# First product of the first MLP by blocks: seven half-width products for eight, in two passes over the chunks

## Chip, cores and metric

One core of one Trainium2 chip. The metric is the device time of one execution in microseconds (us), lower is better. The kernel before ran three times: 810.62, 811.00 and 811.71, median 811.0.

## What is computed

Causal attention with a bias made of running sums, for 4 batches of 8 heads, 576 rows of 64; then two MLPs on 2304 tokens of width 512. All inputs and outputs are float32. The parts that matter here:

```python
x = attention(q, k, v, s)                  # (2304, 512)
h = x @ w_in                               # (2304, 2048)
g = h - np.tanh(h)
x = g @ w_out                              # (2304, 512)
h = x @ w2_in                              # (2304, 1024)
e = np.exp(h - max(h)); solu = h * e / sum(e)
ln = (solu - mean) / np.sqrt(var + 1e-06) * g_ln
out = ln @ w2_out                          # (2304, 512)
```

## The kernel before

Every operand of a matmul is split in a high part (rounded to float32r by ScalarE) and a low part (the rest, by VectorE or GpSimd); a product is three matmuls, high x high, high x low and low x high. Activations lie transposed in xT: features on the partitions, in four tiles kt of 128, tokens along the row. The stages follow each other: attention (16 pairs of heads, in a software pipeline over slots), the first MLP, the second MLP, and each begins while the last one ends.

The first MLP goes over five chunks of tokens: 512, 256 (the short one, c == 1), 512, 512 and 512. Each chunk goes through j = 0 to 15, the 128-wide tiles of the 2048 features. up (L1447) makes one tile of h in a PSUM bank with 4 kt x 3 = 12 matmuls as wide as the chunk; ScalarE takes tanh into gate (L847), VectorE subtracts it from the bank (L1141), ScalarE makes gate_hi (L860), VectorE gate_lo (L1153); down (L1459) adds the tile's part to four PSUM banks y_ps with 12 more matmuls. chunk (L1473) orders ups and downs on TensorE, a down two or four tiles behind its up. gate is a single buffer, gate_hi and gate_lo have two, so step (L843, L1137) waits for earlier downs. The first four ups stand inside the last slots of attention (first_up, L1489), and chunks 2 and 3 are a hardware loop. At a chunk's end copy_y (L977, L1275) brings the four banks to xT, and split_x (L806, L1101) splits the next chunk's x.

w_in and w_out stay in SBUF in both parts after chunk 0, where SP loads them tile by tile through the buffers stage (L549) and ScalarE and VectorE split them between the steps. In the last chunk the same is done for w2_in and w2_out: W2_STEP (L90) and W2O_STEP (L92) are written out by hand and say at which j each part is made, with GpSimd's four sums of w2_in's blocks (L701 to L710) before.

The second MLP already uses the scheme that the change brings to the first. Two token tiles and two halves of the features make a 2 x 2 block matrix; with the sums S1 to S4 of x's blocks and T1 to T4 of the weights' blocks, seven products (PRODUCTS, L94) in three PSUM banks give the four blocks that plain multiplication gives with eight. up2 (L1674) issues them, each 6 matmuls of 512 columns, and waits between them for keep and block_sum (L1296 to L1328), which add what has to be kept from bank to bank; ScalarE's copy_p1 (L1005) keeps the first product. GpSimd makes the sums and parts of x (split_y, L712). Then exp2, solu, moments, shift and normalise turn each row into ln, turn_ln transposes it, and down2 (L1725) multiplies by w2_out, whose parts w2o_hi and w2o_lo carry g_ln.

The order of work on every engine is the order of its program, written out by hand; semaphores count what is done. The end of the first MLP on TensorE is L1754 to L1758:

```python
chunk(NCH - 1, False)
up2(0, 0, 0, {})
down(NCH - 1, FT - 2, False)
down(NCH - 1, FT - 1, False)
up2(1, 1, 1, {4: (0, 0)})
```

## Time and profile before

| | |
|---|---|
| median of three runs | 811.0 us |
| the profiled execution | 810.19 us |
| its span on the core | 808.4 us |
| TensorE busy | 795.9 us, 98% |
| weight loads | 669.5 us, 83% |
| VectorE, ScalarE, GpSimd busy | 58%, 49%, 34% |
| granted TensorE clock | 1.00 |

The span runs from the first to the last instruction of the profile. Matmuls overlap, so the length shown of one (0.39 us at 512 columns) is more than the distance to the next; the distance between starts is what counts. PE is TensorE's matmuls, PEld its weight loads, DVE VectorE, ACT ScalarE, POOL GpSimd.

### The profile page before, as it was taken

The page shows a single profiled execution, that of the slowest core. Times are in us where ns is not written, and L with a number is a line of the kernel's source. Part 1 is how long each engine was busy: PE and PEld are TensorE (multiplying, and loading weights), DVE is VectorE, ACT ScalarE, POOL GpSimd, SP SyncE. Part 2 cuts the span into 40 slices and gives each one's busy share as a digit, 9 for nine tenths or more (in the row PEclk, how much of TensorE's full clock was granted, in tenths as well). Part 3 has the DMA queues.
Part 4 walks back from the last instruction along what each step waited for, and adds up shares of the span by engine and source line. Part 5 has one row for each costly group of instructions (what it writes and reads, how often), then busy time and mean ns, then how long its engine had stood idle before and what let it go on. Part 6 is the DMA issues. An engine that isn't in the chain of part 4 may idle for free. (4 is left out here: it accounts for less than half of the span.)

```text
span 808.4 us, 14647 instructions
## 1 busy us (share of the span) xinstructions
PE 795.9 (98%) x4532; PEld 669.5 (83%) x4532; DVE 465.7 (58%) x1101; ACT 395.9 (49%) x935; POOL 273.7 (34%) x322
## 2 busy tenths in 40 slices
PE   7999999999999999999999999999999999999998
PEld 6888888887888899988888888888887788888886
DVE  5889899897954342422233222453668666666661
ACT  5999999997643232322223222443344344433342
POOL 3778877877100000000000000016553754444400
PEclk9999999999999999999999999999999999999999
DMA  7656556553523200000000000002000000000001
GB/s 182 165 150 157 142 151 160 151 139 115 156 95 103 79 1 1 1 1 1 1 0 0 0 0 0 1 1 104 1 1 0 27 27 27 26 25 14 25 14 53
DMA packets 77723, 46.40 MB, mean 57 GB/s; under 512 B 59824, under 2 KB 68144, under 8 KB 77680
## 3 DMA queue, kind: packets, MB, share of 16 engines
q1 hardware_dynamic: 75232, 45.19, 19.8%
q10 hardware_dynamic: 2448, 0.66, 0.4%
q8 instruction: 24, 0.39, 0.2%
q14 instruction: 19, 0.16, 0.1%
HBM read 40.97 MB, written 4.87 MB: 57 GB/s over the span
## 5 line engine op out<-in xcount | busy, mean ns | idle before, releaser
L1455 PE MATMUL psum<-x_hi,w1i 128*128 128x512 f32 (+1 forms) x640 | 181.9, 369 | 0.5 <-issue 0.5
L1468 PE MATMUL psum<-gate_hi,w1o 128*128 128x512 f32 (+1 forms) x640 | 146.0, 370 | 0.0
L1455 PEld LDWEIGHTS psum<-x_hi,w1i 128*128 128x128 f32 x640 | 115.4, 188 | 21.3 <-issue 0.7
L1468 PEld LDWEIGHTS psum<-gate_hi,w1o 128*128 128x128 f32 x640 | 112.4, 188 | 21.1
L1153 DVE TENSOR_TENSOR gate_lo<-gate,gate_hi 128x512 fp32r<-128x512 f32 (+1 forms) x80 | 53.6, 670 | 125.0 <-ACT gate_hi L860 125.0
L1455 PE MATMUL psum<-x_lo,w1i 128*128 128x512 f32 (+1 forms) x320 | 117.7, 368 | 0.0
L702 POOL TENSOR_TENSOR w2t<-stage 128x512 f32<-128x512 f32 x2 | 4.3, 2154 | 327.9 <-DVE w2x L1127 327.9
L860 ACT ACTIVATE gate_hi<-gate 128x512 fp32r<-128x512 f32 (+1 forms) x80 | 47.2, 590 | 134.6 <-PE psum L1468 126.4
L1141 DVE TENSOR_TENSOR gate<-psum,gate 128x512 f32<-128x512 f32 (+1 forms) x80 | 51.0, 638 | 95.8 <-ACT gate L847 94.2
L847 ACT ACTIVATE gate<-psum 128x512 f32<-128x512 f32 (+1 forms) x80 | 44.4, 555 | 111.8 <-PE psum L1455 90.8
L885 ACT ACTIVATE probs<-probs,neg_max 128x128 f32<-128x128 f32 (+2 forms) x144 | 83.6, 586 | 9.9 <-DVE neg_max L1186 9.7
L1169 DVE TENSOR_TENSOR pT_lo<-psum,pT_hi 128x512 fp32r<-128x512 f32 (+3 forms) x160 | 72.5, 478 | 12.1 <-ACT pT_hi L876 10.7
L1468 PE MATMUL psum<-gate_lo,w1o 128*128 128x512 f32 (+1 forms) x320 | 79.2, 369 | 0.0
L876 ACT ACTIVATE pT_hi<-psum 128x512 fp32r<-128x512 f32 (+3 forms) x160 | 64.1, 434 | 10.4 <-PE psum L1590 9.9
L1455 PEld LDWEIGHTS psum<-x_lo,w1i 128*128 128x128 f32 x320 | 60.2, 188 | 10.1
L1738 PE MATMUL psum<-w2o_a,lnT_hi 128*128 128x512 f32 x216 | 67.8, 395 | 0.3 <-DVE lnT_lo L1379 0.3
L1468 PEld LDWEIGHTS psum<-gate_lo,w1o 128*128 128x128 f32 x320 | 56.9, 189 | 11.1
L1186 DVE CUSTOM_DVE_ANT_0 probs<-psum,cum_bc 128x128 f32<-128x128 f32 (+3 forms) x128 | 58.5, 481 | 11.2 <-PE psum L1518 8.8
L1590 PE MATMUL psum<-ident,probs 128*128 128x128 f32 x400 | 57.9, 275 | 1.0 <-DVE pT_lo L1169 0.5
L1557 PE MATMUL psum<-pT_hi,v_parts 128*128 128x128 f32 (+2 forms) x192 | 56.1, 330 | 0.5 <-DVE pT_lo L1169 0.5
L1705 PE MATMUL psum<-w2x,y_split_a 128*128 128x512 f32 x210 | 50.8, 396 | 0.0
L1557 PE MATMUL psum<-pT_lo,v_parts 128*128 128x128 f32 (+2 forms) x192 | 48.3, 311 | 0.0
(158 smaller groups left out, 1408.5 us busy)
## 6 DMA issues: line engine op xcount, KB each, us to landing
cum_bc<-cum_dram SPq DMA_DIRECT2D x16, 576.0 KB, 4.7
rden_T<-rden_dram SPq DMA_DIRECT2D x32, 144.0 KB, 3.1
out_x<-out_sb SPq DMA_DIRECT2D x18, 256.0 KB, 2.0
stage<-in_q SPq DMA_DIRECT2D x32, 128.0 KB, 2.6
v_raw<-in_v SPq DMA_DIRECT2D x32, 128.0 KB, 3.7
stage<-in_moe_w_in SPq DMA_DIRECT2D x16, 256.0 KB, 3.0
stage<-in_moe_w_out SPq DMA_DIRECT2D x16, 256.0 KB, 3.3
stage<-in_k SPq DMA_DIRECT2D x28, 128.0 KB, 2.3
```

Of the source, the lines that this page charges most:

```text
L876: hi = act.activation(to(pT_hi), ps, ACT.Copy)
L885: act.activation(probs[par][:, at:at + width], probs[par][:, at:at + width], ACT.Exp, bias=neg_max[par][:, col:col + 1], scale=-1.0, accum ...
L1141: dve.tensor_tensor(gate[:, 0:n], h_ps[j % 4][:, 0:n], gate[:, 0:n], ALU.subtract).then_inc(gate_done, 1)
L1153: dve.tensor_tensor(gate_lo[j % 2][:, 0:n], gate[:, 0:n], gate_hi[j % 2][:, 0:n].bitcast(F32), ALU.subtract).then_inc(gate_lo_done, 1)
L1169: lo = dve.tensor_tensor(to(pT_lo), ps, to(pT_hi).bitcast(F32), ALU.subtract)
L1186: dve.tensor_tensor_reduce(probs[par][:, at:at + width], tail_bank(sl) if h is None else score_ps[h][t], cum_tail[:, :] if h is None else ...
L1455: mm = pe.matmul(h_ps[j % 4][:, 0:wide(c)], wp[j][:, kt, :], xp[:, kt, 0:wide(c)], start=(n == 0), stop=(n == 3 * KT - 1))
L1468: mm = pe.matmul(y_ps[m][:, 0:wide(c)], wp[j][:, m * P:(m + 1) * P], gp[j % 2][:, 0:wide(c)], start=(j == 0 and wp is w1o_hi and gp is gat ...
L1557: mm = pe.matmul(x_ps[:, c0:c1], v_parts[par][:, j, 2 * h * D:2 * h * D + P], pp[:, h, j * STEP + c0:j * STEP + c1], start=(j == 0 and n = ...
L1590: mm = pe.transpose(ps[:, n * P:(n + 1) * P], probs[par][:, at:at + P], ident[:, :])
L1705: mm = pe.matmul(h2_ps[n][at], yp[:, of, kt, :], wp[:, kt, :], start=(nth == at and kt == 0 and k == 0), stop=(last and kt == HK - 1 and k ...
L1738: mm = pe.matmul(out_ps[par], lp[par][:, f, :], wp[f][:, :], start=(f == 0 and n == 0), stop=(f == FT2 - 1 and n == 2))
```

## The change

The first MLP runs over half of h (8 of the 16 tiles j, FT1) at a time. CHUNKS lists the passes: chunks 0, 1, 2, 3, 4 with the first half, then 4, 0, 1, 2, 3 with the second. The first pass over chunk 0 is computed as before (8 ups, 8 downs). The other nine runs are 36 groups: a group g is a run and a pair of tiles j, four pairs a run, 28 on full chunks and 8 on the short one (runs 0 and 6). Tokens of the chunk in two halves, features in two halves and the pair's two tiles make the blocks, and products (new) issues seven products of 6 matmuls, each half a chunk wide (n, 256 columns or 128), in banks 0 to 2, with the weights' block as the stationary operand; before it was 24 matmuls of the full width. downs is the old down for the pair's two halves of the gate, one group later.

Beside it: ScalarE copies product 1 and C11 out of PSUM, VectorE adds five block sums per group to h_blocks in SBUF (block_sum1), the tanh and the gate now read h_blocks; before a new chunk seven blocks of x are summed (GpSimd), rounded (ScalarE) and their low parts taken (GpSimd three, VectorE four); each weight pair takes four sums (pair_sums, GpSimd), three copies (pair_hi, 512, 256 and 1024 wide) and three low parts (pair_lo), for the second half in groups 13 to 16, with w_out's in 14 to 17. y of the first pass goes to y_half and by DMA to y_dram, and comes back to be added by GpSimd (add_y); only chunk 4 stays. w2_in is split in the last two groups, w2_out at the start of the second MLP. split_y has 10 instructions in place of 12.

```diff
+    FT1 = FT // 2
+    CHUNKS = [0, 1, 2, 3, 4, 4, 0, 1, 2, 3]
...
+    PAIRS1 = FT1 // 2
+    GROUPS = PAIRS1 * (len(CHUNKS) - 1)
+    LAST_GROUP = GROUPS - 1
...
+        def group(g):
+            run, pair = divmod(g, PAIRS1)
+            return run, pair, wide(CHUNKS[run + 1]) // 2
+        SPLIT_RUNS = [run for run in range(len(CHUNKS) - 1) if CHUNKS[run + 1] != CHUNKS[run]]
+        def ahead_of(g):
+            run, pair = divmod(g + 1, PAIRS1)
+            return run if pair == 0 and run in SPLIT_RUNS else None
+        def x_free(eng, run, name):
+            if run == 0:
+                eng.wait_ge(up_done, FT1 if XB_AT[name] > 2 else AHEAD)
+            else:
+                eng.wait_ge(pair_product, 7 * (PAIRS1 * run - 1) + XB_AT[name] + 1)
...
+            c = CHUNKS[e]
+            return y_half[:, m, 0:wide(c)] if e < NCH else xT[:, m, tokens(c)]
...
+            def store_half(e):
+                sp.wait_ge(y_act, 2 * (e + 1))
+                sp.wait_ge(y_dve, 2 * (e + 1))
+                n = wide(CHUNKS[e])
+                sp.dma_start(y_dram[CHUNKS[e], :, :, 0:n], y_half[:, :, 0:n]).then_inc(y_stored, 16)
...
+                sp.wait_ge(w1i_lo_done, FT1 - 3 + n)
+                sp.wait_ge(w1o_lo_done, FT1 - 3 + n)
+                load_pair(n)
...
+            def pair_sums(n):
...
+                pair_free(pool, n)
+                pool.tensor_tensor(t1, b12, b11, ALU.subtract).then_inc(w1b_summed, 1)
+                pool.tensor_tensor(t3, b22, b12, ALU.subtract).then_inc(w1b_summed, 1)
+                pool.wait_ge(w1b_summed, 4 * n + 1)
+                pool.tensor_tensor(t2, b22, t1, ALU.subtract).then_inc(w1b_summed, 1)
+                pool.wait_ge(w1b_summed, 4 * n + 3)
+                pool.tensor_tensor(t4, b21, t2, ALU.subtract).then_inc(w1b_summed, 1)
...
+            def x_low(run, name):
+                pool.wait_ge(xb_hi_done, 7 * SPLIT_RUNS.index(run) + XB_HI.index(name) + 1)
+                pool.tensor_tensor(x_part(run, name, 1), x_block(run, name), x_part(run, name, 0).bitcast(F32),
+                                   ALU.subtract).then_inc(xb_low_pool, 1)
+            def split_blocks(run):
+                x_low(run, "A11")
+                x_sums(run, XB_SUM)
+                x_low(run, "A12")
+                x_low(run, "A22")
...
-            pool.wait_ge(y_act, 2 * (NCH - 1))
-            pool.wait_ge(y_dve, 2 * (NCH - 1))
-            pool.wait_ge(down_done, FT * (NCH - 1) + 10)
+            pool.wait_ge(x_done, PAIRS)
+            x_sums(0, XB_SUM[:2])
+            pair_sums(0)
+            x_low(0, "A11")
+            pair_sums(1)
+            pair_sums(2)
+            x_sums(0, XB_SUM[2:])
+            x_low(0, "A12")
+            x_low(0, "A22")
+            pair_sums(3)
+            for run in (1, 2, 3):
+                split_blocks(run)
+            for n in range(PAIRS1, 2 * PAIRS1):
+                pair_sums(n)
+            split_blocks(5)
+            add_y(5)
+            split_blocks(6)
+            add_y(6)
+            split_blocks(7)
+            add_y(7)
...
-            pool.wait_ge(up_done, FT * NCH)
+            w2_sums("T1", LAST_GROUP - 2)
+            add_y(8)
+            w2_sums("T2", LAST_GROUP - 1)
+            w2_sums("T4", LAST_GROUP - 1)
...
-            pool.wait_ge(y_act, 2 * NCH)
-            pool.wait_ge(y_dve, 2 * NCH)
...
+            def pair_hi(n):
...
+                hi = w1b[n % PAIRS1][:, 0, :, :, :]
+                pair_free(act, n)
+                act.activation(hi[:, 0:2, :, :], first.rearrange("p (b k) f -> p b k f", b=2), ACT.Copy).then_inc(w1b_hi_done, 1)
+                act.activation(hi[:, 2, :, :], second[:, HK:KT, :], ACT.Copy).then_inc(w1b_hi_done, 1)
+                act.wait_ge(w1b_summed, 4 * (n + 1))
+                act.activation(hi[:, 3:7, :, :], w1b_raw[n % PAIRS1][:, 1, 3:7, :, :], ACT.Copy).then_inc(w1b_hi_done, 1)
...
+                        act.wait_ge(w2_in[kt], 16)
...
+            def copy_first(g):
+                run, pair, n = group(g)
+                act.wait_ge(pair_product, 7 * g + 1)
+                act.wait_ge(gate_done, FT1 + 2 * g)
+                act.activation(h_blocks[:, 1, 0:n], h1_ps[0][:, 0:n], ACT.Copy).then_inc(first_copied, 1)
+            def copy_c11(g):
+                run, pair, n = group(g)
+                act.wait_ge(pair_product, 7 * g + 4)
+                act.activation(h_blocks[:, 0, 0:n], h1_ps[0][:, 0:n], ACT.Copy).then_inc(c11_copied, 1)
+            def tanh(g, t):
+                run, pair, n = group(g)
+                act.wait_ge(block_summed, 5 * g + 4 + t)
+                if t == 1:
+                    act.wait_ge(c11_copied, g + 1)
+                act.wait_ge(gate_lo_done, FT1 + 2 * g + t)
+                act.activation(gate_pair(gate, n), h_pair(t, n), ACT.Tanh).then_inc(tanh_done, 1)
+            def gate_high(g, t):
+                run, pair, n = group(g)
+                u = FT1 + 2 * g + t
                 act.wait_ge(gate_done, u + 1)
...
-                act.activation(gate_hi[j % 2][:, 0:wide(c)], gate[:, 0:wide(c)], ACT.Copy).then_inc(gate_hi_done, 1)
-                if isinstance(c, int) and c == 0 and 0 < j <= FT - AHEAD:
...
+            for g in range(GROUPS):
+                run, pair, n = group(g)
+                ahead = ahead_of(g)
+                copy_first(g)
+                if pair == 1:
+                    copy_y(run)
+                if ahead is not None:
+                    x_hi_part(ahead, "A11")
+                copy_c11(g)
+                if ahead is not None:
+                    x_hi_part(ahead, "S1")
+                if g == 0:
+                    pair_hi(PAIRS1 - 1)
+                if 0 <= g - 3 * PAIRS1 - 1 < PAIRS1:
+                    pair_hi(PAIRS1 + g - 3 * PAIRS1 - 1)
+                if 0 <= g - 3 * PAIRS1 - 2 < PAIRS1:
+                    for j in range(2):
+                        w1o_hi_later(2 * (g - 3 * PAIRS1 - 2) + j)
+                if g == LAST_GROUP - 1:
+                    w2i_hi_part("T1")
+                    w2i_hi_part("T2")
+                    w2i_hi_part("T4")
+                if g == LAST_GROUP:
+                    w2i_hi_part("B11")
+                tanh(g, 0)
+                if ahead is not None:
+                    for name in XB_HI[2:]:
+                        x_hi_part(ahead, name)
+                if g == LAST_GROUP:
+                    w2i_hi_part("B21")
+                    w2i_hi_part("B22")
+                gate_high(g, 0)
+                tanh(g, 1)
+                if g == LAST_GROUP:
...
             def copy_p1(i, n):
                 act.wait_ge(product_done, 7 * i + 1)
                 if isinstance(i, int) and i == 0:
-                    act.wait_ge(w2o_lo_done, 2)
...
+                    act.wait_ge(w2_summed, 4 * HK)
+                    act.wait_ge(w2i_lo_done, 7)
                 wait(act, ln_step, 18 * same_banks(i) - 7)
                 act.activation(h_sums[n][0], h2_ps[n][0], ACT.Copy).then_inc(p1_copied, 1)
...
             copy_p1(0, 0)
+            for f in range(4):
+                w2o_hi_part(f)
             exp2(0, 0, 0)
+            w2o_hi_part(4)
+            w2o_hi_part(5)
             exp2(0, 1, 0)
-            copy_y(NCH - 1)
+            copy_y(len(CHUNKS) - 1)
             normalise(0, 0)
+            w2o_hi_part(6)
+            w2o_hi_part(7)
             copy_p1(1, 1)
...
+            def block_sum1(g, product, at, block):
+                run, pair, n = group(g)
+                dve.wait_ge(pair_product, 7 * g + product)
+                kept = h_blocks[:, 1, 0:n] if block in (1, 2, 3) and product < 4 else h_blocks[:, block, 0:n]
+                dve.tensor_tensor(h_blocks[:, block, 0:n], h1_ps[at][:, 0:n], kept, ALU.add).then_inc(block_summed, 1)
+            def keep_first(g, product, at, block):
+                dve.wait_ge(first_copied, g + 1)
+                block_sum1(g, product, at, block)
...
+            def gate_of(g, t):
+                run, pair, n = group(g)
+                dve.wait_ge(tanh_done, FT1 + 2 * g + t + 1)
+                dve.tensor_tensor(gate_pair(gate, n), h_pair(t, n), gate_pair(gate, n), ALU.subtract).then_inc(gate_done, 1)
...
+            for g in range(GROUPS):
+                run, pair, n = group(g)
+                ahead = ahead_of(g)
+                if pair == 1:
+                    copy_y(run, 2)
+                keep_first(g, 2, 1, 2)
+                keep_first(g, 3, 2, 3)
+                if pair == 1:
+                    copy_y(run, 3)
+                if g == LAST_GROUP - 1:
+                    w2i_lo_part("T1")
+                dve.wait_ge(block_summed, 5 * g + 2)
+                block_sum1(g, 5, 1, 3)
+                block_sum1(g, 6, 2, 2)
+                block_sum1(g, 7, 1, 1)
+                gate_of(g, 0)
+                if ahead is not None:
+                    for name in XB_SUM[:3]:
+                        x_low_sum(ahead, name)
+                if g == LAST_GROUP - 1:
+                    w2i_lo_part("T2")
+                if g == LAST_GROUP:
+                    w2i_lo_part("B11")
+                gate_low(FT1 + 2 * g, 2 * n)
+                if ahead is not None:
+                    x_low_sum(ahead, XB_SUM[3])
+                if g == 0:
+                    pair_lo(PAIRS1 - 1)
+                if 0 <= g - 3 * PAIRS1 - 1 < PAIRS1:
+                    pair_lo(PAIRS1 + g - 3 * PAIRS1 - 1)
+                if g == LAST_GROUP - 1:
+                    w2i_lo_part("T4")
+                if g == LAST_GROUP:
+                    w2i_lo_part("B21")
+                gate_of(g, 1)
+                if 0 <= g - 3 * PAIRS1 - 2 < PAIRS1:
+                    for j in range(2):
+                        w1o_lo_later(2 * (g - 3 * PAIRS1 - 2) + j)
+                if g == LAST_GROUP:
+                    w2i_lo_part("B22")
...
             keep(0, 0)
+            w2o_lo_part(0)
+            w2o_lo_part(1)
             c11(0, 0)
             c22(0, 0)
             c12(0, 0)
             row_max(0, 0)
             c21(0, 0)
             row_max(0, 1)
+            w2o_lo_part(2)
+            w2o_lo_part(3)
             solu(0, 0, 0)
             moments(0, 0)
-            copy_y(NCH - 1)
+            w2o_lo_part(4)
+            w2o_lo_part(5)
+            copy_y(len(CHUNKS) - 1, 2)
+            copy_y(len(CHUNKS) - 1, 3)
             shift(0, 0)
             solu(0, 1, 0)
             keep(1, 1)
             moments(0, 1)
+            w2o_lo_part(6)
...
+            def products(g):
+                run, pair, n = group(g)
+                if run in (0, NCH - 1):
...
+                for nth, (rows, columns, at) in enumerate(PRODUCTS):
+                    if pair == 0 and run in SPLIT_RUNS:
+                        if rows in XB_SUM:
+                            pe.wait_ge(xb_low_dve, 4 * SPLIT_RUNS.index(run) + XB_SUM.index(rows) + 1)
+                        else:
+                            pe.wait_ge(xb_low_pool, 3 * SPLIT_RUNS.index(run) + XB_LOW.index(rows) + 1)
+                    if g == 0 and nth < 3:
+                        pe.wait_ge(gate_done, AHEAD + nth + 1)
+                    elif nth == 0:
+                        pe.wait_ge(c11_copied, g)
+                    elif nth < 3:
+                        pe.wait_ge(block_summed, 5 * g)
+                    elif nth == 3:
+                        pe.wait_ge(first_copied, g + 1)
+                    elif nth < 6:
+                        pe.wait_ge(block_summed, 5 * g + nth - 3)
+                    else:
+                        pe.wait_ge(block_summed, 5 * g + 3)
+                    last = nth == max(k for k, p in enumerate(PRODUCTS) if p[2] == at)
+                    for kt in range(HK):
+                        for k, (xp, wp) in enumerate(((0, hi), (0, lo), (1, hi))):
+                            mm = pe.matmul(h1_ps[at][:, 0:n], wp[:, W1B_AT[columns], kt, :],
+                                           x_blocks[:, XB_AT[rows], xp, kt, 0:n],
+                                           start=(nth == at and kt == 0 and k == 0), stop=(last and kt == HK - 1 and k == 2),
+                                           skip_group_check=True)
+                    mm.then_inc(pair_product, 1)
+            def downs(g):
+                run, pair, n = group(g)
...
+                    pe.wait_ge(y_act, 2 * (run + 1))
+                    pe.wait_ge(y_dve, 2 * (run + 1))
+                for t in range(2):
+                    if run == NCH - 1:
+                        pe.wait_ge(w1o_lo_done, FT1 + 2 * pair + t + 1)
+                    down(FT1 + 2 * g + t, 2 * pair + t, pair == 0 and t == 0, pair == PAIRS1 - 1 and t == 1, 2 * n)
             def first_up(j):
...
+                first_down(j)
+            products(0)
+            first_down(FT1 - 1)
+            for g in range(1, GROUPS):
+                products(g)
+                downs(g - 1)
...
             up2(0, 0, 0, {})
-            down(NCH - 1, FT - 2, False)
-            down(NCH - 1, FT - 1, False)
+            downs(LAST_GROUP)
             up2(1, 1, 1, {4: (0, 0)})
```

## Rows read from the trace of the kernel before

**Rows 1.** The page: busy time, share of the span, instructions.
```profile
PE 795.9 (98%) x4532; PEld 669.5 (83%) x4532; DVE 465.7 (58%) x1101; ACT 395.9 (49%) x935; POOL 273.7 (34%) x322
```
**Rows 2.** Chunks 2 to 4: length, busy PE, PEld, DVE, ACT, POOL; PEclk, DMA, GB/s.
```profile
336.83:580.00 243.17, 243.17 (x1066) 199.69 (x1065) 84.33 (x117) 72.93 (x115) 21.55 (x14) 1.00 0.03 9
```
**Rows 3.** Timeline (start us, length us): first matmuls of ups, chunks 0 and 1.
```profile
222.62 0.62 PE L1455 MATMUL psum<-x_hi,w1i 128*128 128x512 f32 x2
...
228.11 0.62 PE L1455 MATMUL psum<-x_hi,w1i 128*128 128x512 f32 x2
...
299.79 0.40 PE L1455 MATMUL psum<-x_hi,w1i 128*128 128x256 f32 x2
...
302.64 0.40 PE L1455 MATMUL psum<-x_hi,w1i 128*128 128x256 f32 x2
```
**Rows 4.** Timeline, TensorE: narrow matmuls in attention, transposes in the second MLP.
```profile
186.86 0.25 PE L1557 MATMUL psum<-pT_hi,v_parts 128*128 128x192 f32 x1
...
187.22 0.55 PE L1590 MATMUL psum<-ident,probs 128*128 128x128 f32 x3
...
616.85 1.03 PE L1721 MATMUL psum<-ident,act 128*128 128x128 f32 x8
617.64 3.25 PE L1705 MATMUL psum<-w2x,y_split_b 128*128 128x512 f32 x12
```
**Rows 5.** Timeline, weight loads beside the same matmuls of attention.
```profile
186.97 0.19 PEld L1557 LDWEIGHTS psum<-pT_hi,v_parts 128*128 128x128 f32 x1
187.08 0.19 PEld L1557 LDWEIGHTS psum<-pT_lo,v_parts 128*128 128x128 f32 x1
```
**Rows 6.** Timeline: from TensorE to VectorE and from VectorE to TensorE.
```profile
594.77 9.96 PE L1705 MATMUL psum<-w2x,y_split_a 128*128 128x512 f32 x42
...
597.84 0.69 DVE L1301 TENSOR_TENSOR stage<-psum,stage 128x512 f32<-128x512 f32 x1 [0.57 <-PE psum L1705]
...
189.47 0.69 DVE L1169 TENSOR_TENSOR pT_lo<-psum,pT_hi 128x512 fp32r<-128x512 f32 x1
...
190.31 0.56 PE L1557 MATMUL psum<-pT_hi,v_parts 128*128 128x128 f32 x2 [0.54 <-DVE pT_lo L1169]
```
**Rows 7.** Groups of instructions by form, and two rows of the timeline (they begin with a time).
```profile
L847 ACT ACTIVATE gate<-psum 128x512 f32<-128x512 f32 x64 | 38.3, 598 | 98.3 <-PE psum L1455 78.4 <-DVE gate_lo L1153 19.9
...
L980 ACT ACTIVATE xT<-psum 128x256 f32<-128x256 f32 x2 | 0.7, 381 | 0.3 <-PE psum L1468 0.3
...
L825 ACT ACTIVATE w2x<-w2t 128x1024 fp32r<-128x1024 f32 x4 | 4.2, 1050 | 0.0
...
L832 ACT ACTIVATE w2x<-stage 128x512 fp32r<-128x512 f32 x6 | 7.0, 1214 | 0.0
...
L1141 DVE TENSOR_TENSOR gate<-psum,gate 128x256 f32<-128x256 f32 x16 | 6.8, 424 | 13.0 <-ACT gate L847 13.0
...
L1127 DVE TENSOR_TENSOR w2x<-stage,w2x 128x512 fp32r<-128x512 f32 x6 | 6.6, 1158 | 4.6 <-ACT w2x L832 4.6
...
L1133 DVE SCALAR_TENSOR_TENSOR w2o_a<-stage,g_col,w2o_a 128x512 fp32r<-128x512 f32 x6 | 4.5, 804 | 0.0
...
L734 POOL TENSOR_TENSOR y_split_b<-y_sum,y_split_b 128x512 fp32r<-128x512 f32 x4 | 5.2, 1297 | 0.7 <-POOL y_split_b L731 0.7
...
560.83 1.22 DVE L1122 TENSOR_TENSOR w2x<-w2t,w2x 128x1024 fp32r<-128x1024 f32 x1 [0.26 <-ACT w2x L825]
...
245.52 0.69 DVE L1153 TENSOR_TENSOR gate_lo<-gate,gate_hi 128x512 fp32r<-128x512 f32 x1 [2.79 <-ACT gate_hi L860]
```
**Rows 8.** Timeline, VectorE's gate_lo while GpSimd forms w2_in's sums (542.5 to 558.1).
```profile
542.50 4.28 POOL L702 TENSOR_TENSOR w2t<-stage 128x512 f32<-128x512 f32 x2 [327.91 <-DVE w2x L1127]
...
546.26 1.07 DVE L1153 TENSOR_TENSOR gate_lo<-gate,gate_hi 128x512 fp32r<-128x512 f32 x1 [1.91 <-ACT gate_hi L860]
...
551.75 0.86 DVE L1153 TENSOR_TENSOR gate_lo<-gate,gate_hi 128x512 fp32r<-128x512 f32 x1 [2.17 <-ACT gate_hi L860]
...
557.24 1.39 DVE L1153 TENSOR_TENSOR gate_lo<-gate,gate_hi 128x512 fp32r<-128x512 f32 x1 [2.17 <-ACT gate_hi L860]
```

559 lines of the change are left out of this document (338 added, 221 removed).

## The prediction

> **What bounds the kernel now.** I read the page first: TensorE is busy for 98% of the span [rows 1]. Then the table of stretches: in the steady chunks of the first MLP it is busy in every microsecond, while ScalarE and VectorE work a third of the time and GpSimd hardly at all [rows 2]. So here the time is the pitch of the matmuls, and I took that from the timeline: 24 matmuls of 512 columns from 222.62 to 228.11, 5.49 us or 0.2288 each; 24 of 256 columns from 299.79 to 302.64, 2.85 us or 0.1188 each [rows 3]. A line through both is 0.0088 us + 0.00043 us per column. Then I asked what a matmul costs whose columns are few: in attention four of 192, 192, 64 and 64 columns take 0.36 us where the line gives 0.25, and the eight 128-column transposes take 0.79, where it gives 0.51 [rows 4]; the weight loads beside them follow each other at 0.11 [rows 5]. Weights in 32 bits seem to need 0.11 us each, and 256 columns just cover that.
>
> **Matmuls removed and added.** For a pair of feature tiles the first product was 24 matmuls of a chunk's width; now it is 42 of half that width. A group on a full chunk: 24 x 0.2288 = 5.49 becomes 42 x 0.1188 = 4.99, -0.50; 28 groups give **-14.1 us**. A group on the short chunk (256 tokens) now has 128 columns: 24 x 0.1188 = 2.85 becomes 42 x p. The line gives p = 0.064; the eight transposes need 0.79/8 = 0.099, the first load having run ahead [rows 4]; the loads' own pitch is 0.11 [rows 5]. I take 0.11, since 42 matmuls in a row each bring fresh weights and only the first load can run ahead: 4.62, +1.77; 8 groups give **+14.2 us** (ends: -1.4 by the line, +14.2; 10.5 at 0.099). The gain and this loss cancel. The second products and the eight first ups and downs are unchanged in number.
>
> The loads' pitch in the trace is 0.11 us [rows 5]. The Trainium skill (TensorE: Matmul & The Clock Gate, "Back-to-back issue gap") gives about 81 ns for a sustained matmul of 128 columns, its weight load included; by that p would be 0.081, a short group +0.55, and this term +4.4. No row here shows such a pitch with float32 weights.
>
> **Hand-offs.** The rest is waits, which the old stream had none of. Prices: the length shown of a matmul is 0.39 at 512 columns and 0.28 at 256 (0.62 - 0.23 and 0.40 - 0.12 [rows 3]). VectorE starts 0.1 after that end (597.84, after 594.77 + 11 x 0.233 + 0.39), and a matmul 0.15 after VectorE's (190.31, after 189.47 + 0.69) [rows 6]. ScalarE needs 0.60 for 512 elements, 0.38 for 256, 1.05 for 1024, 1.21 for a strided 512; VectorE 0.42 for 256, 0.69 for 512, 1.22 for 1024, 1.16 strided, 0.80 for a scaled w2_out tile; GpSimd 1.30 for 512 [rows 7]. I walked the in-order queues with these, S being the start of a group's products.
>
> - *Seventh product.* It waits for the sum of the fifth. The fifth's last matmul starts at S+3.44 and shows at +3.82; the sum ends at 4.24, the matmul can start at 4.39, and was due at 4.28: 0.04 to 0.12, I take 0.09; 0.04 in short groups. 28 x 0.09 + 8 x 0.04 = **+2.8**. Otherwise a plain group closes: gate_hi of the second half waits for the previous group's second down (S+10.6), ends at 11.6, the copy of P1 ends at 12.0, and the fourth product, due at 12.7, finds it (P1: the group's first product).
> - *Start.* Count from the first down; ups and downs take 2.75, so products(0) is due at 30.2. ScalarE's gate_hi(5) waits for down 3 (19.6), then pair_hi(0) to 22.1, VectorE's pair_lo(0) to 23.4 and gate(6) to 24.1; gate_hi(6) waits for down 4 (25.0), pair_hi(1) to 27.6, pair_lo(1) to 28.9, gate(7) 29.6, gate_hi(7) 30.3, pair_lo(2) to 33.5, and only then x_low of S2, 33.9. The second product, due at 30.9, starts at 34.0: 3.0. pair_hi(3) and pair_lo(3) in group 0 and y's copies put the P1 copy of group 1 1.0 late and its sums 0.5. **+4.5**.
> - *New chunk.* In the group ahead of six split runs ScalarE has seven more copies of 512, VectorE four more lows, GpSimd seven operations of 1.3. GpSimd's chain (low of A11, S1, S2, S4, S3) starts at S+2.1 and ends at 8.9; the copy of S3 at 9.6 stands before gate_hi(g,0), 1.5 later than its down allows; through gate_lo, the low of S3, tanh, gate and gate_hi the P1 copy of the next group ends at 13.5, its fourth product was due at 12.7: 0.9, four times. Ahead of groups 4 and 28 the group is short (due at 9.55, copy at 12.3): 2.8, twice. **+9.2**. The short chunk's own parts (256 wide) fit.
> - *VectorE beside GpSimd.* While GpSimd formed w2's sums, gate_lo, whose two inputs are in SBUF, took 1.07 and 1.39 [rows 8] instead of 0.69 [rows 7]. The gate, now from h_blocks, has both inputs in SBUF too. The mean stretch of three is (0.38 + 0.17 + 0.70)/3 = 0.42; with two such operations on each of the six late chains **+5.0** (ends 0 and 6 x 5 x 0.7 = 21).
>  The Trainium skill (SBUF — State Buffer, the bullets on the shared port pair) calls their common port an exclusive lock held for a whole instruction; by that rule the stretch is up to a GpSimd operation, 1.3, and the upper end would be 39. The trace agrees that they hinder each other, with 0.70 as its longest.
> - *Weights of the second pass* (groups 13 to 17). pair_hi hides before tanh, but pair_lo (2.2) stands between gate_lo and gate(g,1): P1's copy 0.7 late; with w1o's two lows the next sums 0.5 more in three groups. 0.7 + 3 x 1.2 = **+4.3**. y's copies in each run's second group: **+0.5**.
> - *Groups 34 and 35.* w2's T1 low stands before the fifth sum, and waits for ScalarE's T1 copy (4.5): it ends at 5.8, the seventh product starts at 6.35, not 4.28: **+2.1**. In group 35 ScalarE has B21 and B22 (four strided copies, released by the last product at S+5.4) before gate_hi: it frees at 11.4; gate_lo 12.1, B21 low 14.2, gate 14.9, B22 low 17.0, gate_lo 17.7, T3 low 18.9, and copy_p1(0), which waits for that, 19.6. up2(0) starts at 10.6 and its fourth product is due at 10.6 + 18 x 0.233 = 14.8: **+4.9**.
> - *First tiles of the second MLP.* w2_out's eight copies and lows moved here. From the end of up2(0): solu and moments to 6.2, lows 4 and 5 to 7.7, y's copies 8.9, shift 9.4, normalise 10.7, copies 6 and 7 11.9, copy_p1(1) 12.5; the fourth product of up2(1) is due at 5.5 + 4.2 = 9.65: 2.9. Lows 6 and 7 put c22 and c11 before its seventh product 1.75 late, and ln_lo the first output 0.35. **+5.0**.
>
> Each of these waits can be half as long, since an engine's next operation may start up to 0.1 before the end shown of the last, or half as long again where GpSimd is in the way.
>
> At nothing: y's trip through DRAM and the weights' second loads (DMA moves 9 GB/s in the steady chunks [rows 2] and each has a run of 42 us; cover gone, one group shows a gap), GpSimd's add_y (4 x 1.3 in a run; if late, split_y of a later tile pair), unrolled groups in place of a loop (chunk 1 is unrolled now, without a gap [rows 3]), fewer waits in split_y, which runs a tile pair ahead. In SP's queue y's stores wait for the copies and stand before the second pass's w_out, which is needed 4 runs later. The granted clock is 1.00 [rows 2], full speed (2.4 GHz), and I charge nothing for it.
>
> Sum of waits 2.8 + 4.5 + 9.2 + 5.0 + 4.3 + 0.5 + 2.1 + 4.9 + 5.0 = 38.3; with -14.1 + 14.2: +38.4. The profiled execution took 810.2 (span 808.4 and 1.8 around it), so 848.6; the median 811.0 is 0.8 above it. I say **849**.
>
> **Rivals.**
> 1. *Weight loads partly hidden.* The four attention matmuls come at 0.09 each although two have 64 columns. Then a short group is 42 x 0.09 = 3.78, +0.93: 7.4 in place of 14.2, **842**. Against it: two of them have 192 columns, and the loads had run ahead. By the Trainium skill's 81 ns (above) it would be 839.
> 2. *Short groups by the line.* The 128-column pitch is 0.064, as if transposes alone were slow: -1.4 in place of 14.2, **833**. Against it: the loads of f32r weights in rows 5.
> 3. *Slack eats the waits.* My walk adds lengths, and back to back the engines start up to 0.1 earlier than the length; over chains of ten that is half of the stall. Waits 19: **830**. For it: ScalarE and VectorE have a third of their time used.
> 4. *Faster: the columns count everywhere.* TensorE's column saving is -14.1 - 1.4 = -15.5, in all 36 groups. It decides as soon as the waits sum to less than 15.5. With a quarter of mine (9.6) it is **804**. Against it: the +4.9 and the start alone are 9.4, and both are fixed by the order of the queues.
> 5. *The change does not save columns*: excluded by the loops (42 for 48 halves). That all of it balances within 0.2% is chance only.
>
> **Numbers.** Forecast 0.50, rivals 1 to 4 have 0.15, 0.15, 0.10, 0.07, balance 0.03. A measurement tells 0.2% (1.6 us) from no change. Faster 0.07, same 0.03, slower 0.90. Range: below, rivals 2 and 3 together (849 - 16 - 19 = 814); above, the lock at 0.7 on four operations of each chain (+12) and 2 at the ends, 862.
>
> **What would show it.** In the changed profile: full groups with 42 matmuls in 5.0 us and short ones in 4.6 (2.7 for rival 2, 3.8 for rival 1); a gap of 0.1 before each seventh product; gaps before the second product of group 0, the fourth of groups 4, 8, 12, 20, 28 and 32, of groups 14 to 17, the seventh of 34, the fourth of up2(0) and of up2(1). I am wrong if TensorE's idle time in the first MLP stays under 10 us, or if the short groups take under 3 us.

## The result, and the profile after

The changed kernel takes 895.65 us (892.34 to 897.98), the kernel before 811.21 beside it: a ratio of 1.104, 95% interval 1.100 to 1.108. Slower, as forecast, but by 84.4 us in place of 38, and outside the range (814 to 862). Its profiled execution has a span of 894.8, and its four runs spread over 5.6 us, so that differences of 2 or 3 us from it mean little. The page of the changed kernel (busy time with share of the span and instructions, then the slices of section 2), against [rows 1]:

```profile
PE 831.0 (93%) x5180; PEld 723.3 (81%) x5180; DVE 612.3 (68%) x1323; ACT 453.7 (51%) x1073; POOL 400.0 (45%) x397
...
PE   7999999999988999989998999797877799999998
PEclk9999999999979999999998997899997999999999
```

Two things are new against the page of before. VectorE gained 147 us of busy time for 222 more instructions. And the granted clock dips, where the page of before has a 9 in all 40 slices:

```profile
PEclk9999999999999999999999999999999999999999
```

The stretches of the changed kernel show where (length, busy PE, PEld, DVE, ACT, POOL, then PEclk, DMA share, GB/s):

```profile
196.16:725.76 529.60, 478.20 (x2800) 425.47 (x2801) 342.05 (x547) 213.88 (x417) 187.32 (x144) 0.94 0.12 40
...
250.32:257.35 7.03, 7.03 (x36) 7.03 (x37) 2.77 (x6) 2.46 (x5) 3.70 (x5) 0.56 0.22 75
262.05:266.68 4.63, 4.63 (x43) 4.63 (x42) 2.70 (x7) 2.09 (x6) 0.00 (x0) 1.00 0.48 170
...
336.94:341.30 4.36, 4.36 (x25) 4.29 (x25) 1.83 (x5) 0.57 (x2) 0.00 (x0) 0.66 0.00 0
...
541.30:546.48 5.18, 5.18 (x24) 5.18 (x25) 1.22 (x5) 0.69 (x2) 0.00 (x0) 0.50 0.08 26
546.48:551.63 5.15, 5.15 (x25) 5.15 (x26) 1.48 (x4) 0.83 (x2) 0.00 (x0) 0.51 0.00 0
```

262.05 to 266.68 is a short group: 42 matmuls in 4.63 us, the 0.11 forecast. The others each stand behind a pause of TensorE: 42 matmuls less six at 250.32, behind 3.19 us, take 7.03 us at a clock of 0.56, the 24 behind 2.87 us at 336.94 take 4.36 and not the 3.0 of a plain group; a pause of only 1.03 us at 540.3, among short groups, is followed by over 10 us at 0.50, the lower level (1.2 GHz). The timeline around group 8, the first full chunk change, shows how such a pause comes about (start, length, and in brackets the idle time ahead with its releaser):

```profile
331.79 2.28 PE L1881 MATMUL psum<-x_blocks,w1b_a 128*128 128x256 f32 x18
336.94 4.52 PE L1881 MATMUL psum<-x_blocks,w1b_a 128*128 128x256 f32 x24 [2.87 <-ACT h_blocks L1107]
...
328.71 1.73 POOL L870 TENSOR_TENSOR x_raw<-xT 128x512 f32<-128x512 f32 x1
330.40 3.44 POOL L875 TENSOR_TENSOR x_blocks<-xT,x_blocks 128x512 fp32r<-128x512 f32 x2
...
327.51 5.18 DVE L1411 TENSOR_TENSOR x_blocks<-x_raw,x_blocks 128x512 fp32r<-128x512 f32 x3
332.61 1.78 DVE L1470 TENSOR_TENSOR gate_lo<-gate,gate_hi 128x512 fp32r<-128x512 f32 x1
334.31 0.68 DVE L1411 TENSOR_TENSOR x_blocks<-x_raw,x_blocks 128x512 fp32r<-128x512 f32 x1
```

The chain is the forecast one (late lows, gate_lo, tanh, gate, gate_hi, copy of P1), but VectorE's three lows take 5.18 us where three cost 1.9, and gate_lo 1.78 where it costs 0.69 [rows 7], up to 334.4, 0.55 us past the end of GpSimd's last instruction; the very next one, with GpSimd idle, takes 0.68. The plainest case is in a short group, the gate of group 25 beside the addition of y:

```profile
533.85 4.60 POOL L891 TENSOR_TENSOR xT<-xT,y_half 128x2048 f32<-128x2048 f32 x1 [16.09 <-issue]
...
535.64 3.09 DVE L1488 TENSOR_TENSOR gate<-h_blocks,gate 128x256 f32<-128x256 f32 x1
```

0.42 us of work took 3.09: it ended 0.3 after GpSimd's single instruction did (538.45). The pause of group 26 follows, with the 24 matmuls behind it, where a plain full group has its 42 from 310.53 to 315.69, in 5.16 us:

```profile
541.30 5.38 PE L1881 MATMUL psum<-x_blocks,w1b_b 128*128 128x128 f32 x24 [1.03 <-ACT h_blocks L1107]
...
310.53 5.32 PE L1881 MATMUL psum<-x_blocks,w1b_b 128*128 128x256 f32 x42
315.69 2.01 PE L1843 MATMUL psum<-gate_hi,w1o 128*128 128x512 f32 x8
```

**The sum.** From the first up to the turn ahead of up2(3) (638.73 in the kernel before) the changed kernel needs 529.6 us and the kernel before 443.3, 86.3 more. TensorE's idle time there is 51.4 against 1.2: 50.2 more. How the other 36 divide is for the experiments. The stretch of the kernel before:

```profile
195.47:638.73 443.26, 442.10 (x2152) 371.22 (x2153) 195.85 (x325) 156.12 (x279) 59.60 (x58) 1.00 0.09 27
```

### The profile page after: what moved, and what is told of

It reads as the page before. It is cut to its first block, busy times and chain, and to the rows that moved or that the text cites. A ratio compares the mean times of both kernels' runs of the same rounds, so it can differ in the third digit from the quotient of the medians.

```text
span 894.8 us, 16487 instructions
## 1 busy us (share of the span) xinstructions
PE 831.0 (93%) x5180; PEld 723.3 (81%) x5180; DVE 612.3 (68%) x1323; ACT 453.7 (51%) x1073; POOL 400.0 (45%) x397
## 3 DMA queue, kind: packets, MB, share of 16 engines
q1 hardware_dynamic: 77584, 54.63, 20.8%
HBM read 46.74 MB, written 8.54 MB: 62 GB/s over the span
## 4 chain that ended last, share of the span: by engine, by line
PE 70%; DVE 16%; issue 6%; ACT 4%; POOL 1%; DMA 0%; SPq 0%; DVEq 0%; POOLq 0%; ACTq 0%
PE psum L1881 17%; PE psum L1843 14%; PE psum L2155 9%; PE psum L2122 8%; PE psum L1965 6%; PE psum L1922 4%; PE psum L1998 4%; DVE x_blocks L1411 4%; DVE gate_lo L1470 3%; DVE gate L1488 3%; PE psum L1834 2%; PE psum L2016 2%; PE psum L2138 1%; PE psum L1940 1%; PE psum L1926 1%
## 5 line engine op out<-in xcount | busy, mean ns | idle before, releaser
L1881 PE MATMUL psum<-x_blocks,w1b_a 128*128 128x256 f32 (+1 forms) x756 | 110.4, 307 | 28.6 <-ACT h_blocks L1107 21.5
L1881 PEld LDWEIGHTS psum<-x_blocks,w1b_a 128*128 128x128 f32 x756 | 105.4, 215 | 34.2 <-issue 19.7
L875 POOL TENSOR_TENSOR x_blocks<-xT,x_blocks 128x512 fp32r<-128x512 f32 (+1 forms) x24 | 34.1, 1434 | 190.7 <-ACT x_blocks L1064 190.7
L1478 DVE TENSOR_TENSOR h_blocks<-psum,h_blocks 128x256 f32<-128x256 f32 (+1 forms) x180 | 69.0, 393 | 71.0 <-PE psum L1881 70.9
L2155 PE MATMUL psum<-w2o,lnT 128*128 128x512 f32 x432 | 103.2, 395 | 0.0
L1881 PE MATMUL psum<-x_blocks,w1b_b 128*128 128x256 f32 (+1 forms) x756 | 98.0, 288 | 4.3 <-ACT h_blocks L1107 2.7
L1881 PEld LDWEIGHTS psum<-x_blocks,w1b_b 128*128 128x128 f32 x756 | 95.1, 195 | 7.8 <-ACT h_blocks L1107 3.5
L2155 PEld LDWEIGHTS psum<-w2o,lnT 128*128 128x128 f32 x432 | 80.9, 189 | 17.1 <-issue 0.4
L1120 ACT ACTIVATE gate<-h_blocks 128x512 f32<-128x512 f32 (+1 forms) x72 | 41.9, 582 | 87.0 <-DVE gate_lo L1470 44.2
L1488 DVE TENSOR_TENSOR gate<-h_blocks,gate 128x512 f32<-128x512 f32 (+1 forms) x72 | 60.4, 839 | 20.0 <-ACT gate L1120 19.9
```

The lines of the kernel that those rows point to most:

```text
L1478: dve.tensor_tensor(h_blocks[:, block, 0:n], h1_ps[at][:, 0:n], kept, ALU.add).then_inc(block_summed, 1)
L1488: dve.tensor_tensor(gate_pair(gate, n), h_pair(t, n), gate_pair(gate, n), ALU.subtract).then_inc(gate_done, 1)
L1881: mm = pe.matmul(h1_ps[at][:, 0:n], wp[:, W1B_AT[columns], kt, :], x_blocks[:, XB_AT[rows], xp, kt, 0:n], start=(nth == at and kt == 0 and ...
L2155: mm = pe.matmul(out_ps[par], lp[par][:, f, :], wp[f][:, :], start=(f == 0 and n == 0), stop=(f == FT2 - 1 and n == 2))
```

## The experiments

Two theories stand for the excess. **A**: each pause leaves the granted clock at half, and TensorE pays behind it. **B**: a VectorE instruction with both inputs in SBUF waits until GpSimd's running instruction has ended. **C** is the pitch floor of the weight loads, as predicted. The rival to A and B is the prediction's own picture: order of the queues, and a stretch of at most 0.7.

### The single costs, measured behind the kernel before

```diff
+ for k in range(6): 48 matmuls of 512 columns; wait for ScalarE's copies (128, 512, 1024, 2048, 2 x 2048 elements, 128)
+ for n in (512, 256, 192, 160, 128, 64): 48 float32r matmuls of n columns, fresh weights each
+ beside the first: VectorE 6 x (SBUF, SBUF), 6 x (PSUM, SBUF), 3 x 256 wide, 4 x; GpSimd 12 and 10 x 512, 2 x 2048, 8 copies
```

> The kernel before, with measurements of single costs behind its last matmul; its own work is unchanged, 808 us up to there. (1) Pitch: rows of 48 float32r matmuls with fresh weights and 512, 256, 192, 160, 128 and 64 columns, then 48 bf16 ones of 128. If a float32r weight load sets a floor of 0.11 us: 0.229, 0.119, 0.11, 0.11, 0.11, 0.11. If the line through 512 and 256 columns holds below: 0.229, 0.119, 0.091, 0.078, 0.064, 0.036. (2) Clock: six rows of 48 matmuls of 512 columns (11.0 us each at 1.00), between them TensorE waits for ScalarE's copies of 128, 512, 1024, 2048 and twice 2048 elements, idle for about 0.5, 1, 1.5, 2.5 and 4.5 us. Theory A, the clock follows what TensorE did just before: behind idle times over 1 us the next matmuls are at 0.5 for some us, pitch 0.43, and behind the shortest not. Rival, the low clock in the changed kernel has another cause: all at 1.00. (3) The port: VectorE's subtractions with both inputs in SBUF, 512 wide, 0.69 us alone. Theory B, one of them waits until GpSimd's running instruction has ended: beside GpSimd's of 512 (1.3 us) one comes every 1.7 to 2 us; the first 256-wide one beside a GpSimd instruction of 2048 elements (4.6 us) takes up to 5 us; with an input from PSUM 0.69 as alone. The prediction's reading: stretched by 0.42, never more than 0.7, so 1.1 and at most 1.4 us; the 256-wide ones 0.8 to 1.1.

The stretches of that run (columns as above) are the rows of 256, 192, 160, 128 and 64 columns, each of 48 matmuls, the last one cut where its clock changes; ahead of them the rows behind pauses of 0.63 and 4.18 us:

```profile
817.30:828.66 11.36, 11.36 (x48) 8.94 (x48) 0.00 (x0) 0.00 (x0) 0.00 (x0) 1.00 0.00 0
...
871.40:884.40 13.00, 12.93 (x48) 10.07 (x48) 2.85 (x4) 0.02 (x1) 5.40 (x8) 0.87 0.00 0
...
896.24:901.95 5.71, 5.71 (x49) 5.71 (x48) 0.00 (x0) 0.00 (x0) 0.00 (x0) 1.00 0.01 3
901.95:907.29 5.34, 5.34 (x50) 5.34 (x49) 0.00 (x0) 0.00 (x0) 0.00 (x0) 1.00 0.00 0
907.29:912.64 5.35, 5.35 (x51) 5.35 (x49) 0.00 (x0) 0.00 (x0) 0.00 (x0) 1.00 0.00 0
912.64:917.98 5.34, 5.34 (x50) 5.34 (x50) 0.00 (x0) 0.00 (x0) 0.00 (x0) 1.00 0.01 3
917.98:919.74 1.76, 1.76 (x19) 1.76 (x18) 0.00 (x0) 0.00 (x0) 0.00 (x0) 1.00 0.00 0
919.74:926.16 6.42, 6.42 (x34) 6.42 (x34) 0.00 (x0) 0.00 (x0) 0.00 (x0) 0.53 0.00 0
```

C holds: 5.71/48 = 0.119 at 256 columns, and 5.34/48 = 0.111 at 192, 160 and 128 alike. The matmuls of 64 columns start 0.111 apart too, and 0.213 once the clock has fallen; 48 in bf16 with 128 columns, behind them, come at 0.056 at full clock, so the floor belongs to the float32r ones. A holds in part: behind dense rows of 512 columns pauses of 0.63, 0.95, 1.38 and 2.23 us left the clock at 1.00, against my "over 1 us"; only the one of 4.18 brought it down, for 1.6 us of extra time. But in the row of 64 columns it fell with no pause at all. So the pause alone does not decide. Narrow matmuls stood ahead of the fall here and ahead of the pause of group 26; what it takes is not settled by these rows.

B holds. VectorE's groups by form in the second and third stretch, one of two SBUF inputs and one with an input from PSUM, GpSimd running beside both:

```profile
L1469 DVE TENSOR_TENSOR stage<-act,act 128x512 f32<-128x512 f32 x6 | 9.8, 1689 | 0.0
...
L1469 DVE TENSOR_TENSOR stage<-psum,act 128x512 f32<-128x512 f32 x6 | 3.7, 682 | 0.0
```

1.69 us each against 0.68. The 256-wide ones came too early for the long instructions; beside GpSimd's of 512 they took 1.50 each, over the 1.1 of the rival. One of 512 met the end of the second long one (timeline):

```profile
861.22 9.24 POOL L804 TENSOR_TENSOR xT<-w2x 128x2048 f32<-128x2048 f32 x2 [0.17 <-POOL xT L804]
...
868.01 2.99 DVE L1469 TENSOR_TENSOR stage<-act,act 128x512 f32<-128x512 f32 x1
```

It ended at 871.00, 0.54 after GpSimd did. The 512-wide ones all end so: the gate_lo of group 8 0.55 after GpSimd's instruction, and all of the first six here 0.55 after, that is 0.14 less than their own 0.69. The three behind it, beside GpSimd's plain copies of 0.83, took 1.09 each.

### Filling the pauses

```diff
+ FILL = {(0, 1): 26, (4, 3): 27, (8, 3): 23, (12, 3): 23, (20, 3): 23, (26, 3): 8, (28, 3): 26, (32, 3): 28, "up2": 38}
+ for k in range(count): pe.matmul(bank(3)[...], weights, moving, start=True, stop=True)   # ahead of that wait
```

> The changed kernel, with matmuls that compute nothing wanted put where TensorE stood still for over 1 us: 26 before the second product of group 0, 27, 23, 23, 23, 8, 26 and 28 before the fourth product of groups 4, 8, 12, 20, 26, 28 and 32, 38 of 512 columns before the fourth of up2(0). They fit into the idle times seen, so no wait of another engine is changed. Theory A (a stand leaves the granted clock at half, and TensorE pays for it behind the stand): all that ran at 0.5 to 0.66 comes back: 5.0 at group 0, 1.6, 1.5, 1.6, 2.8, 4.8, 2.8 and 1.5 at the seven others, 2.7 at up2(0), together 24; 895.7 becomes 872, somewhat more (up to 880) where a quicker group meets a wait that the slow one hid. Rival (the clock falls for a reason outside TensorE's own pauses, or costs nothing because the waits would end as late): within 2 us of 895.7, with the low clock still there.

Measured 877.31 (ratio to the kernel before 1.083, 1.081 to 1.085), 18.3 less. The mean granted clock rose from 0.966 to 0.998. The matmuls behind the first pause, and those behind the pause of group 8, with the whole stretch to the same turn as above (columns as above):

```profile
250.13:254.27 4.14, 4.14 (x37) 4.14 (x37) 2.67 (x6) 1.43 (x4) 3.70 (x5) 1.00 0.39 127
331.88:335.06 3.18, 3.18 (x25) 2.99 (x25) 1.83 (x5) 0.67 (x2) 0.00 (x0) 1.00 0.00 0
...
196.16:705.49 509.33, 486.38 (x3023) 432.08 (x3022) 340.48 (x547) 213.32 (x416) 188.00 (x144) 1.00 0.12 42
```

7.03 became 4.14, 4.36 became 3.18. That more matmuls make the kernel faster decides for A. In 29.9 us of the 486.4 busy only fills run, which leaves 456.5; the changed kernel's own matmuls took 478.2, so **the lower clock cost it some 22 us** (21.7; a short stretch at half clock behind 696.5 is left, which can add up to 1.7). This stretch of the program is 20.3 us shorter (529.6 less 509.3), since idle time and fills together are 1.4 more than the idle time was: some fills outlasted their pause, and group 1, faster now, meets two waits (0.56 and 0.21) that the slow clock had hidden. And 86.3 - 50.2 - 21.7 leaves 14.4 that is not shown as idle time. As an estimate from the rows, 5.1 of it are 0.16 for each of 32 more pauses, since a pause is shown only from the end shown of a matmul and not from when the next was due, and 4.8 the seventh products (below); the rest, 4.5, is open.

The same pause did not always cost the same. In the changed kernel the 24 matmuls behind the 2.87 us of groups 8, 12 and 20 took 4.36, 4.43 and 5.26 us, and in the next section a run has the 3.22 us pause of group 28 with no half clock behind it.

### Two places where GpSimd is beside VectorE

```diff
  w2_sums("T3", LAST_GROUP + 1)
+ pool.wait_ge(w2i_lo_done, 7)
  split_y(1, 1)
```

> The changed kernel with one wait more: GpSimd begins the split of y's second tile pair only when VectorE has made the last of w2_in's low parts (T3). Theory B (VectorE's instructions with both inputs in SBUF stand until GpSimd's has ended): from GpSimd's last sum (659.6) on VectorE's chain runs at its own lengths, 0.69 for gate_lo and gate, 2.2 for two strided lows, 1.22 for T3: its last low ends near 668.3, not 674.8, the idle time before up2(0)'s fourth product falls from 9.2 to about 2.8, and the clock behind it is less low; the split itself, some 12 us undisturbed, still ends near 680, before up2(1). Together 7 to 9 us: 887 to 889. Rival (the order of the queues sets it, as the prediction had it for 4.9, and the rest is the slow clock): the idle time stays over 7, and the total within 3 us of 895.7, or grows, if the later split is what up2(1) then waits for.

Measured 888.19 (1.095, 1.092 to 1.098), 7.5 less. VectorE's chain (timeline), with GpSimd waiting from 658.6 on, then TensorE's pause in this run, and the same pause in the changed kernel:

```profile
660.39 0.67 DVE L1471 TENSOR_TENSOR gate_lo<-gate,gate_hi 128x512 fp32r<-128x512 f32 x1
660.98 2.25 DVE L1449 TENSOR_TENSOR w2x_b<-stage,w2x_b 128x512 fp32r<-128x512 f32 x2
663.13 0.70 DVE L1489 TENSOR_TENSOR gate<-h_blocks,gate 128x512 f32<-128x512 f32 x1
663.72 2.20 DVE L1449 TENSOR_TENSOR w2x_c<-stage,w2x_c 128x512 fp32r<-128x512 f32 x2
665.79 0.73 DVE L1471 TENSOR_TENSOR gate_lo<-gate,gate_hi 128x512 fp32r<-128x512 f32 x1
666.39 1.27 DVE L1412 TENSOR_TENSOR w2x_b<-w2b_raw,w2x_b 128x1024 fp32r<-128x1024 f32 x1
...
668.42 0.73 PE L2123 MATMUL psum<-w2x_b,y_hi 128*128 128x512 f32 x2 [3.44 <-ACT stage L1304]
...
675.52 1.22 PE L2122 MATMUL psum<-w2x_b,y_hi 128*128 128x512 f32 x2 [9.19 <-ACT stage L1303]
```

The last low ends at 667.7, not 674.8, and the pause before up2(0)'s fourth product is 3.44, not 9.19. A wait added to GpSimd makes the kernel faster: B, and not the order of the queues, made most of that pause.

```diff
- pool.tensor_tensor(own, own, y_half[:, :, 0:wide(c)], ALU.add).then_inc(y_added, 1)
+ for m in range(KT): ins = pool.tensor_tensor(xT[:, m, tokens(c)], xT[:, m, tokens(c)], y_half[:, m, 0:wide(c)], ALU.add)
```

> The changed kernel with GpSimd's addition of a chunk's y (one instruction of 2048 elements, 4.6 us) cut into four of 512. Theory B: in group 25 VectorE's gate, 256 wide, took 3.09 us because it began 2.8 us before that long instruction ended; with four short ones it waits for one at most, 1.7 us, the fourth product of group 26 is not late, its idle time of 1.03 us is gone, and with it (theory A) the half clock behind it, 2.5 + 2.3 us: 889.8, 5.9 less. Rival (stretching by bandwidth, so that the same bytes stretch it as much): gate still near 3 us, total within 1.5 us of 895.7.

Measured 883.66 (1.090, 1.088 to 1.092), 12.0 less, twice the forecast. The gate of group 25 takes 1.01, the pause at group 26 is gone and group 26's products and downs take 4.77 and 2.92, not 8.33 and 5.15:

```profile
533.57 5.38 POOL L892 TENSOR_TENSOR xT<-xT,y_half 128x512 f32<-128x512 f32 x4 [16.09 <-issue]
...
535.37 1.01 DVE L1490 TENSOR_TENSOR gate<-h_blocks,gate 128x256 f32<-128x256 f32 x1
```

The rest is elsewhere: group 28 with its downs 2.4 less (its pause of 3.22 us is there, but its clock is 1.00 now), groups 33 and 34 1.7 less, beside the addition of chunk 2, and 2.8 behind up2(1), where the clock stayed up. The same bytes in shorter instructions hinder less, which a sharing of bandwidth would not give.

### The change of chunk

```diff
+ w = 8 if run > 1 else wide(CHUNKS[run + 1]) // 2      # of 256 columns: lows of A11, A12, A22 on GpSimd
```

This leaves out most of three low parts of x from group 8 on; it is a measurement and no cure.

> The changed kernel; of the three low parts of x that GpSimd makes ahead of each new chunk (A11, A12, A22) only 8 of 256 columns are made, from group 8 on; the boundary at group 4 is left whole, as a control. Theory B (the port is held for a whole GpSimd instruction): ahead of group 8 GpSimd's last two instructions (330.4 to 333.8) are what held VectorE's lows and gate_lo (1.78 for 0.69); without them gate_lo takes 0.69 again, two of the three lows come at 0.6, the copy of P1 ends near 334.0, when the fourth product is due: idle 0 to 0.3 in place of 2.87 at groups 8, 12 and 20, under 1 at 28 and 32, still 3.2 at 4, and no half clock behind those that are gone: 895.7 - 17 - 7 = 872, at most 876. Rival (VectorE's own queue is too full there, with four lows in it, whatever GpSimd does): the idle times stay over 1.5 at groups 8, 12 and 20, 885 or more.

Measured 874.33 (1.078, 1.076 to 1.079), 21.3 less. Timeline, VectorE and TensorE at group 8:

```profile
328.30 3.04 DVE L1412 TENSOR_TENSOR x_blocks<-x_raw,x_blocks 128x512 fp32r<-128x512 f32 x3
331.26 0.68 DVE L1471 TENSOR_TENSOR gate_lo<-gate,gate_hi 128x512 fp32r<-128x512 f32 x1
...
334.50 3.35 PE L1882 MATMUL psum<-x_blocks,w1b_a 128*128 128x256 f32 x24 [0.33 <-ACT h_blocks L1108]
```

2.87 became 0.33, and group 4, the control, keeps 3.21. 1.15 and 2.08 are left at 28 and 32, over the forecast. Then the same work moved to VectorE, with nothing left out:

```diff
- x_low(run, "A12"); x_low(run, "A22")                  # GpSimd
+ x_low_block(ahead, "A12")                             # VectorE, behind the low of S3
+ x_low_block(ahead, "A22")                             # VectorE, behind gate_of(g, 1)
```

> The changed kernel with the low parts of A12 and A22 made by VectorE in place of GpSimd, behind the low of S3 and behind the second gate; no work is left out and VectorE has two instructions of 0.6 us more at each new chunk. Theory B: what VectorE lost there was not its own work but GpSimd's instructions; it gains more by their absence (3.2 us) than it pays (1.2). The copy of P1 ends about 0.5 later than in the run with narrow lows: idle time before the fourth product 0.3 to 0.7 at groups 8, 12 and 20, 1.5 at 4 and 28, 2.3 at 32, no half clock behind the first three: 874 to 879. Rival (VectorE's queue is what is full at a new chunk): the idle times stay at 2.9 or grow, 895 to 900.

Measured 879.45 (1.086, 1.084 to 1.087), 16.2 less and just above the forecast: giving VectorE more work shortened its chain. The pauses are 1.16 to 1.19 at groups 8, 12 and 20, over the forecast; at groups 0 and 32 they grew (4.57 from 3.19, 4.12 from 3.55). Group 8:

```profile
334.71 3.34 PE L1891 MATMUL psum<-x_blocks,w1b_a 128*128 128x256 f32 x24 [1.18 <-ACT h_blocks L1104]
```

A cure by order alone:

```diff
- act.activation(h_blocks[:, 1, 0:n], h1_ps[0][:, 0:n], ACT.Copy)   # behind gate_high(g - 1, 1)
+ act.activation(first_kept[:, 0:n], h1_ps[0][:, 0:n], ACT.Copy)    # at a chunk change ahead of tanh(g - 1, 1)
```

> The changed kernel with a buffer of its own for the copy of P1 and, at the eight groups that begin a new chunk, that copy moved ahead of the tanh and gate_hi of the previous group's second half, and the sums of the second and third products ahead of its gate. No work is taken away, the port is as busy. If the 2.9 to 3.5 us of idle time at groups 4, 8, 12, 20, 28 and 32 come from the place of that copy at the end of the late chain, they go: what is left is the fifth product waiting for the sums, which now follow VectorE's gate_lo and the low of S3, 0.8 each; 18.6 - 4.8 = 13.8 less idle time and, with theory A, 9 less at half clock: 872. Rival (the late chain itself is what TensorE needs next, so the wait only moves to the second products, which need gate_lo): the same idle time stands at the down matmuls of those groups, total within 3 us of 895.7.

Measured 882.85 (1.088, 1.087 to 1.090), 12.8 less, where 23 were expected. At groups 8, 12 and 20 the pause before the fourth product went; two others came, before the fifth (0.72) and the seventh product (1.04), since VectorE now has the held-up gate and gate_lo between the fifth product and its sum. So 1.76 of the 2.87 had only moved. Group 24, which paused nowhere before, pauses 0.73 and loses some 2.5 us with the half clock behind it.

### The chunk widths

```diff
- return SHORT if c == 1 else CH                        # 512, 256, 512, 512, 512
+ return CH if c == 0 else (TOK - CH) // (NCH - 1)      # 512, 448, 448, 448, 448
```

> The changed kernel with other chunk widths: 512 tokens and four times 448, in place of four times 512 and 256. If the weight loads' 0.11 us is the floor of a first product's pitch (theory C), the eight short groups cost 4.63 each for half the columns; now 32 groups have 224 columns at 0.112, 4.85 with the hand-off, and 4 have 256, 5.16: 175.8 in place of 181.5, 5.7 less. The second products have the same columns in as many chunks. With the short groups the idle time and half clock of group 26 (5.8) and the longer waits at groups 4 and 28 go, some 3 more: 895.7 becomes 880 to 882. Rival (the first product's time goes by columns, the short groups are slow for another reason, for instance their waits): the groups of 448 take 42 x 0.105 = 4.4 and the total falls under 870. If the slightly shorter groups only find later copies: 888 or more.

Measured 885.64 (1.092, 1.090 to 1.094), 10.0 less. A group of 448 takes 4.83 for its first product, as theory C says (42 x 0.111 and the hand-off), so 6 of the ten is the floor of the pitch (28 x 5.16 + 8 x 4.64 become 32 x 4.83 + 4 x 5.16). It fell 4 to 6 short. In its profile the second product of group 0 waits 4.70, in place of 3.19, and groups 1 and 24, which paused nowhere before, pause 1.46 and 2.08; with the lower clock behind these their first products take 7.84 and 8.54 us. But this profile is of its slowest execution (890.53, the other four took 884.8 to 885.9, at a clock of 0.979 in place of 0.969), so it shows more of the low clock than the median has.

### All cures together

```diff
+ the addition of y in pieces, the held split of y, the early copy of P1 (the three edits above)
```

> The changed kernel with three cures at once and no work left out: the early copy of P1 in its own buffer, the addition of y in four pieces, and the split of y's second tile pair held until w2_in's lows are made. The pieces gave 12.0 less and the held split 7.5 (measured), the early copy is expected to give 23; at different places, so they add: 895.7 - 42.5 = 853. If theory A and B hold, no stretch of half clock is left but at group 0 and before up2(0)'s fourth product, and the idle time of the first MLP is under 17 us of the 46 now. Still over the 811 of the kernel before: the short chunk's 14, the first group's 8 and the start of the second MLP's 15 are untouched. If the cures share one cause they give less together, 860 to 870.

Measured 870.48 (1.072, 1.070 to 1.074), 17 over the forecast: the early copy gives 10 less than it was booked with, and of the 32.3 that the three gave alone 25.2 came.

```diff
+ the addition in pieces, the held split, the lows of A12 and A22 on VectorE, the even chunks (edits above)
```

> All cures that measured well, with no work left out: chunks of 512 and four times 448, the lows of A12 and A22 on VectorE, the addition of y in four pieces, the split of the second tile pair held. Each alone from 895.7: 15 (even chunks, expected, of which 5.8 at group 26 is the same as in the pieces), 19 (lows on VectorE, expected), 12.0 (pieces, measured), 7.5 (held split, measured). Without what is counted twice: 895.7 - 15 - 19 - 12 - 7.5 + 6 = 848, between 843 and 855. The kernel before (811) stays ahead: the first product of all chunks now saves TensorE 6 to 7 us against it, and the first group (8 of idle time and half clock), the weights' second pass (3) and the start of the second MLP (15) cost more than that.

Measured 863.10 (1.065, 1.063 to 1.067), 15 over. Alone the four gave 45.7; less the 6 of group 26 that two of them share 39.7; 32.6 came. What the rest overlaps in is not settled.

```diff
+ the four above; FILL = {(0, 1): 27, (20, 3): 10, (32, 3): 24, "up2": 13}; runs 0 and 8 keep their lows on GpSimd
```

> The run with all cures and even chunks, with two things more: matmuls that compute nothing wanted fill the idle times left before the second product of group 0 (27), before the fourth of groups 20 (10) and 32 (24) and of up2(0) (13 of 512 columns), and at the first and the last chunk change the lows of A12 and A22 go back to GpSimd, since VectorE's two extra instructions lengthened the idle time there (4.6 in place of 3.2 at group 0, 4.1 in place of 3.6 at 32). Its mean granted clock was 0.986 over a span of 861, so half clock still cost it about 12 us. Theory A: the clock goes to 0.99 or more, 863.1 - 9 - 2 (the shorter idle times) + 1 (waits that a faster group meets) = 853, between 850 and 858. Rival: a fill that outlasts the wait it stands in costs as much as it brings, 860 or more.

Measured 858.25 (1.059, 1.057 to 1.061), just above the forecast, and the best version of the change: 37.4 less than it, 47.5 more than the kernel before, at a mean granted clock of 0.998 in the profiled execution and 0.994 to 0.996 in the others. TensorE still has 27.6 us of pauses between the first up and 700 us, and 9.8 in which only fills run. No experiment made the change pay; even with no pause at all the first products would take TensorE 7 us less than before with even chunks (4 x 4.99 + 32 x 42 x 0.1113 = 169.6, against 28 x 5.49 + 8 x 2.85 = 176.5), and as long as before with the short one. With the hand-offs as measured (5.16 and 4.83 a group) they take 175.2, and 1.3 of the 7 is left.

## Why the prediction was wrong

Pauses stand in all the places that the prediction named, so its walk through the queues held; what failed is two prices. Idle times are those shown, of the changed kernel.

- **Full and short groups** (-14.1, +14.2): right. 42 matmuls in 4.63 to 4.64 in short groups; rivals 1 and 2 (0.09, 0.064) are refuted by the flat 0.111 from 192 to 128 columns. The Trainium skill's 81 ns for 128 columns (TensorE: Matmul & The Clock Gate, "Back-to-back issue gap") does not hold for these float32r weights: the row shows 0.111.
- **Seventh product** (+2.8): plain groups take 5.16, so 0.17 each over 4.99, 4.8 for 28.
- **Start** (+4.5): the second product of group 0 waits 3.19, forecast 3.0. The wait of group 1 was hidden by the slow clock; with the pause filled it is 0.77, forecast 1.5.
- **New chunk, and VectorE beside GpSimd** (9.2 + 5.0 = 14.2): the places are right, group 24 shows nothing, as forecast, but the sum is 20.8, and 1.15 at groups 5 and 29. **The failed step is "the mean stretch of three is 0.42", with 0.70 as the longest.** It is no stretch: gate_lo began at 546.26 and GpSimd's instruction ended at 546.78 [rows 8]; 0.52 of waiting and the work's own 0.69, less the 0.14 of all such cases, are the 1.07 seen. The other two fit as well: GpSimd's instructions ended at 552.06 and 558.08, 0.31 and 0.84 after VectorE's began, and these took 0.86 and 1.39. Those rows showed how late VectorE had come in GpSimd's instruction, not the most that it can lose. The Trainium skill (SBUF — State Buffer, "Who interferes with whom") says it: a lock for a whole instruction. The runs agree, 1.69 in place of 0.68 beside GpSimd's instructions of 1.57. I had it in the text and let three samples bound it.
- **add_y "at nothing"** failed for the same reason: 1.03 of idle time at group 26 and 4.8 lost at half clock behind it; cut in pieces it gave back 12.0 in all.
- **Second pass** (4.3 + 0.5): 2.3 at groups 14 to 17, half, as rival 3 had it.
- **Groups 33 to 35** (2.1 + 4.9): 1.92 and 2.50 at 33 and 34, 1.50 ahead of up2(0), 9.19 in it. Those at 33 and ahead of up2(0) were not forecast. In up2(0) the order was right; the lows held up by w2_in's last sums and split_y (3.2 to 4.2 for a pair that costs 2.2) are most of the rest, since 3.44 was left when split_y waited.
- **First tiles of the second MLP** (+5.0): 6.7 less the 1.1 of before, 5.6. 1.10 before the fifth up was not forecast.
- **"The granted clock is 1.00, and I charge nothing for it"** is the second failed step. That row [rows 2] is of a TensorE without pauses; the prediction has 38 us of them. The lower clock cost some 22 us, more than any wait of mine.

So waits and hand-offs made 64.6 (50.2 + 14.4) where 38.3 were forecast, and the clock some 22 where nothing was: of the miss of 48, 22 is clock and 26 waits. How much of the 26 is the port is not measured as one sum; the pauses that went with GpSimd's work are 5.8 in up2(0) and 2.5 at each of groups 8, 12 and 20. Rival 4 and a zero change were never near. The upper end should have held the lock at its own 39 in place of the 12 that I took, less the 5.0 already in the sum; that gives 885, still under the 895.7 measured: it takes the clock as well.

## What to carry to other kernels

A change that puts pauses of a few us into a dense stream of matmuls must be charged twice: for the pause, and for the matmuls behind it at half clock (here some 22 for 51, from nothing to 5 us a pause). A row that shows two engines hindering each other gives one sample of a wait; read the other engine's instruction beside it, and price the whole of it. Before work is moved to an idle GpSimd, ask which VectorE instructions with two SBUF inputs run beside it: here VectorE did the same work itself and the kernel became 16 us faster.

## What was unexpected of the hardware

The granted clock fell in a row of 64-column matmuls with no pause (0.53 from 919.74 on), and stayed at 1.00 behind pauses of up to 2.23 us in dense 512-column rows; behind 128-column groups 1.03 us was enough for over 10 us at 0.50. One GpSimd instruction of 4.60 us held a VectorE instruction of 0.42 for 3.09; beside GpSimd's 512-wide subtractions two SBUF inputs took 1.69, and one from PSUM 0.68, its time alone. GpSimd pays too: its 512-wide subtractions took 1.57 on the mean in that stretch, 1.29 beside the PSUM ones. And 48 float32r matmuls take 5.34 us with 128 columns as with 192, while in bf16 those of 128 columns come 0.056 apart.
